# Attention of a fused kernel: the turns of queries and results through three PSUM banks in another order

## What is computed

```python
def phi(x):
    proj = np.einsum('bhsd,md->bhsm', x, omega)
    h = proj - np.sum(x * x, axis=-1, keepdims=True) / 2.0
    h = h - np.max(h, axis=-1, keepdims=True)
    return np.exp(h) / np.sqrt(m)
q_p, k_p = phi(q * scale), phi(k * scale)          # 4 x 8 heads, 576 x 128 each
kv = np.einsum('bhsm,bhsd->bhmd', k_p, v)
z = np.sum(k_p, axis=2)
num = np.einsum('bhsm,bhmd->bhsd', q_p, kv)
den = np.einsum('bhsm,bhm->bhs', q_p, z)[..., None] + 1e-06
attn_out = num / den
```

## Time and profile before

| | |
|---|---|
| median of 3 runs | 805.19 us (804.8 to 805.69) |
| profiled execution | 807.05 us, its span 805.2 us |
| TensorE, VectorE, ScalarE, GpSimd busy | 96%, 44%, 38%, 40% of the span |
| granted TensorE clock, mean | 0.992 |
| attention | the first 157 us |

### The profile page before, as it was taken

The page is one execution under the profiler, slowest core; times in us unless marked ns, Lnnn a source line. Parts: engine busy times, 40 slices in busy tenths (PEclk is TensorE's granted clock), DMA queues, the critical chain, the costliest instruction groups (busy, mean ns, idle before and its releaser), DMA issues.

```text
span 805.2 us, 15805 instructions
## 1 busy us (share of the span) xinstructions
PE 774.9 (96%) x5510; PEld 712.5 (88%) x5511; DVE 356.6 (44%) x908; ACT 308.9 (38%) x714; POOL 322.7 (40%) x280
## 2 busy tenths in 40 slices
PE   8899889999999999999999999999999999999994
PEld 7777778799899989988989998997999999999994
DVE  5777767511224424433442444666762322332221
ACT  3777776633232242232223224263224324425220
POOL 6777886135222222222222223243026726627421
PEclk9999999999999999999999999999999999999998
DMA  7876774011050020020002001141062532611111
GB/s 269 296 273 231 246 266 154 19 35 53 9 176 1 0 78 0 0 75 3 0 0 78 0 0 40 44 186 36 15 238 60 175 132 65 214 57 39 29 59 31
DMA packets 25732, 74.17 MB, mean 92 GB/s; under 512 B 3152, under 2 KB 4048, under 8 KB 25568
## 3 DMA queue, kind: packets, MB, share of 16 engines
q1 hardware_dynamic: 22432, 63.68, 22.7%
q0 software_dynamic: 3264, 10.03, 4.1%
HBM read 61.11 MB, written 12.58 MB: 92 GB/s over the span
## 4 chain that ended last, share of the span: by engine, by line
PE 88%; ACT 4%; DVE 3%; issue 3%; DMA 0%; ACTq 0%; POOL 0%; SPq 0%; POOLq 0%; DVEq 0%
PE pj L712 25%; PE nm L894 16%; PE pj L1312 8%; PE kv L894 8%; PE kv L1328 6%; PE nm L1328 6%; PE nm L1312 5%; PE pj L264 3%; PE kv L282 3%; ACT feat L427 2%; PE pj L1341 1%; PE tr L1299 1%; PE kv L313 1%; PE nm L340 1%; DVE pj L514 1%
## 5 line engine op out<-in xcount | busy, mean ns | idle before, releaser
L868 POOL TENSOR_TENSOR gl<-g,gh 128x384 fp32r<-128x384 f32 x96 | 100.9, 1053 | 304.7 <-ACT gh L730 304.7
L725 DVE TENSOR_TENSOR g<-pj,sg 128x384 f32<-128x384 f32 x96 | 53.5, 557 | 222.7 <-ACT sg L720 222.4
L720 ACT ACTIVATE sg<-pj 128x384 f32<-128x384 f32 x96 | 47.2, 491 | 253.3 <-PE pj L712 253.3
L712 PE MATMUL pj<-xh,win_h 128*128 128x384 f32 x384 | 129.6, 337 | 1.3 <-DVE xl L747 1.3
L712 PE MATMUL pj<-xh,win_l 128*128 128x384 f32 x384 | 129.5, 337 | 0.0
L712 PE MATMUL pj<-xl,win_h 128*128 128x384 f32 x384 | 129.0, 336 | 0.0
L712 PEld LDWEIGHTS pj<-xh,win_h 128*128 128x128 f32 x384 | 72.2, 188 | 5.2 <-DVE xl L747 1.5
L712 PEld LDWEIGHTS pj<-xl,win_h 128*128 128x128 f32 x384 | 72.1, 188 | 3.6
L712 PEld LDWEIGHTS pj<-xh,win_l 128*128 128x128 f32 x384 | 72.1, 188 | 0.0
L1312 PE MATMUL pj<-xTh,W 128*128 128x288 f32 x320 | 71.1, 302 | 0.0
L836 DVE SCALAR_TENSOR_TENSOR raw<-tr,xT 128x512 f32<-128x512 f32 x90 | 58.6, 688 | 8.2 <-DVE g L725 7.6
(11 more groups left out here) (255 smaller groups left out, 1691.1 us busy)
## 6 DMA issues: line engine op xcount, KB each, us to landing
wraw<-in_moe_w SPq DMA_DIRECT2D x7, 2048.0 KB, 10.8
ve<-in_v_z SPq DMA_DIRECT2D x16, 585.0 KB, 3.8
qk<-in_qk_n SPq DMA_DIRECT2D x15, 576.0 KB, 6.0
qkT<-in_qk_t SPq DMA_DIRECT2D x15, 576.0 KB, 6.8
y_rows<-ys SPq DMA_DIRECT2D x18, 256.0 KB, 2.4
stage<-in_moe_w_in SPq DMA_DIRECT2D x8, 512.0 KB, 7.1
y_early<-ys SPq DMA_DIRECT2D x12, 256.0 KB, 2.7
stage<-in_moe_w_out SPq DMA_DIRECT2D x4, 512.0 KB, 6.6
```

The costliest lines, as they stand in the source:

```text
L712: mm = eng.matmul(ph[f % 3][:, 0:BT], w[f // F1A][:, c, f % F1A, :], x[:, c, :], start=(c == 0 and w is win_h and x is xh), stop=(c == DC ...
L725: eng.tensor_tensor(g32[f % 2][:, :], ph[f % 3][:, 0:BT], sg[f % 2][:, :], ALU.mult).then_inc(v_g, 1)
L868: eng.tensor_tensor(gl[f % 3][:, :], g32[f % 2][:, :], gh[f % 3][:, :].bitcast(F32), ALU.subtract).then_inc(g_gl, 1)
```

## The change

The second query turn of each step goes into nm0, in all steps, and stands straight after the first, ahead of the third projection. The second result turn goes into nm1. The third query turn stands between the first and the second result turn. Waits follow the banks: the turn into nm0 waits for VectorE's quotient out of it, output 1 waits for the copy out of nm1, the sums no longer wait for a query copy. On ScalarE the exponentials b of group 1 move ahead of the copies of the result turns and of the third query turn, and the exponentials a of group 0 move from behind `copy_kv` to behind those copies: in even steps behind the exponentials b of group 2, just ahead of the other two a.

```diff
--- before.py
+++ after.py
@@ -276,27 +276,25 @@
             need(eng, a_kv, i)
             if a == 1 and not (isinstance(i, int) and i == 1):
                 need(eng, a_xs, 3 * n)
-            else:
-                need(eng, a_qf, 3 * i - 1)
             for j in range(RJ):
                 mm = eng.matmul(kv[:, 0:VW], feat[a][:, j, :], ve[a][:, j, :],
                                 start=(j == 0), stop=(j == RJ - 1))
             mm.then_inc(p_kv, 1)
 
-        def turn_qf(i, n, a, g, before):
+        def turn_qf(i, n, a, g):
 
             if g == 1:
                 eng.wait_ge(a_exa, PG * i + 3)
             else:
                 eng.wait_ge(a_exb, PG * i + 2 + g // 2)
 
-            if before or g == 0:
-                need(eng, a_qf, 3 * i + g)
+            if g == 0:
+                need(eng, a_qf, 3 * i)
             elif g == 1:
-                eng.wait_ge(a_kv, i + 1)
+                need(eng, v_nm, OG * (i - 1) + 1)
             else:
                 eng.wait_ge(a_qf, 3 * i + 1)
-            bank = kv if g == 1 and not before else tr
+            bank = nm[0] if g == 1 else tr
             for j in range(3):
                 mm = eng.transpose(bank[:, j * P:(j + 1) * P], feat[a][:, RJ + 3 * g + j, :], ident[:, :])
             mm.then_inc(t_qf, 1)
@@ -304,13 +302,14 @@
         def turn_x(n, g, unit):
 
 
+
             if g == 0:
                 eng.wait_ge(v_nm, 2 * OG * (n + 1))
                 eng.wait_ge(a_kv, unit + 1)
-            else:
-                eng.wait_ge(a_xs, 3 * n + g)
+            elif g == 2:
+                eng.wait_ge(a_xs, 3 * n + 1)
             for j in range(3):
-                mm = eng.transpose(kv[:, j * P:(j + 1) * P],
+                mm = eng.transpose((nm[1] if g == 1 else kv)[:, j * P:(j + 1) * P],
                                    xs[:, 3 * g + j, :, :].rearrange("p h d -> p (h d)"), ident[:, :])
             mm.then_inc(t_xs, 1)
 
@@ -327,13 +326,16 @@
                                    xs[:, 3 * g + j, :, :].rearrange("p h d -> p (h d)"), ident[:, :])
             mm.then_inc(t_xs, 1)
 
-        def output(i, n, a, t):
+        def output(i, n, a, t, before=False):
 
 
             lo, hi = O_GROUPS[t]
             eng.wait_ge(a_qf, 3 * i + (hi + 2) // 3)
             if t == 0:
                 eng.wait_ge(a_kv, i + 1)
+            elif before:
+
+                need(eng, a_xs, 3 * n - 1)
             need(eng, v_nm, OG * (i - 1) + t + 1)
             for j in range(lo, hi):
                 for b in range(2):
@@ -361,10 +363,10 @@
             before = a == 0 and not (isinstance(i, int) and i == 0)
             if last:
                 sums(i, n, a)
-                turn_qf(i, n, a, 0, before)
+                turn_qf(i, n, a, 0)
                 dense["up"](eng, 0, 0, (v_sb, PG * UNITS - 1))
-                turn_qf(i, n, a, 1, before)
-                turn_qf(i, n, a, 2, before)
+                turn_qf(i, n, a, 1)
+                turn_qf(i, n, a, 2)
                 dense["up"](eng, 0, 1, (a_exb, PG * UNITS - 1))
                 output(i, n, a, 0)
                 output(i, n, a, 1)
@@ -373,27 +375,28 @@
                     turn_last(g)
                 return
 
+
             project(*x, 0)
             project(*x, 1)
             sums(i, n, a)
-            turn_qf(i, n, a, 0, before)
+            turn_qf(i, n, a, 0)
+            turn_qf(i, n, a, 1)
             project(*x, 2)
             if before:
                 turn_x(n - 1, 0, i)
-            turn_qf(i, n, a, 1, before)
+            turn_qf(i, n, a, 2)
             if before:
                 turn_x(n - 1, 1, i)
-            turn_qf(i, n, a, 2, before)
-            if before:
                 turn_x(n - 1, 2, i)
             output(i, n, a, 0)
-            output(i, n, a, 1)
+            output(i, n, a, 1, before)
 
         half_steps(eng, step)
 
     def scalar(eng):
-        def copy_x(n, g, bank=kv):
-
+        def copy_x(n, g, bank=None):
+
+            bank = bank if bank is not None else nm[1] if g == 1 else kv
             eng.wait_ge(t_xs, 3 * n + g + 1)
             at = xT[:, :].rearrange("p (e b j c t) -> p e c j b t", e=2, b=2, j=RJ, c=DC)
             eng.activation(at[:, bass.ds(n // DC, 1), bass.ds(n % DC, 1), 3 * g:3 * g + 3, :, :]
@@ -401,9 +404,9 @@
                            bank[:, 0:3 * P].rearrange("p (j b t) -> p j b t", b=2, t=HD),
                            ACT.Copy).then_inc(a_xs, 1)
 
-        def copy_qf(i, n, a, g, before):
+        def copy_qf(i, n, a, g):
             eng.wait_ge(t_qf, 3 * i + g + 1)
-            bank = kv if g == 1 and not before else tr
+            bank = nm[0] if g == 1 else tr
             eng.activation(qfT[:, 3 * g:3 * g + 3, :].rearrange("p t c -> p (t c)"),
                            bank[:, 0:3 * P], ACT.Copy).then_inc(a_qf, 1)
 
@@ -439,10 +442,10 @@
             before = a == 0 and not (isinstance(i, int) and i == 0)
             if last:
                 copy_kv(i, n, a)
-                copy_qf(i, n, a, 0, before)
+                copy_qf(i, n, a, 0)
                 dense["sig"](eng, 0, 0)
-                copy_qf(i, n, a, 1, before)
-                copy_qf(i, n, a, 2, before)
+                copy_qf(i, n, a, 1)
+                copy_qf(i, n, a, 2)
                 dense["high"](eng, 0, 0)
                 dense["sig"](eng, 0, 1)
                 dense["high"](eng, 0, 1)
@@ -452,26 +455,26 @@
                 return
             exps_b(*x, 0)
             copy_kv(i, n, a)
-            exps_a(*x, 0)
-            copy_qf(i, n, a, 0, before)
+            copy_qf(i, n, a, 0)
+            copy_qf(i, n, a, 1)
+            exps_b(*x, 1)
             if before:
                 copy_x(n - 1, 0)
-            copy_qf(i, n, a, 1, before)
+            copy_qf(i, n, a, 2)
             if before:
                 copy_x(n - 1, 1)
-                copy_qf(i, n, a, 2, before)
-            exps_b(*x, 1)
-            if before:
                 copy_x(n - 1, 2)
             else:
-                copy_qf(i, n, a, 2, before)
-            exps_a(*x, 1)
+                exps_a(*x, 0)
             if isinstance(i, int) and i == UNITS - 2:
 
                 eng.wait_ge(g_sq, 4 * i)
                 eng.wait_ge(g_wl, NWIN + NWO)
                 dense["split_h"](eng, 0, 0)
             exps_b(*x, 2)
+            if before:
+                exps_a(*x, 0)
+            exps_a(*x, 1)
             exps_a(*x, 2)
             if isinstance(i, int) and i == UNITS - 2:
                 dense["split_h"](eng, 0, 1)
```

## The result

The changed kernel took 792.83 us in the median of 4 runs (790.65 to 793.36), the kernel before beside it 805.0 us (802.6 to 805.69): a ratio of 0.9849, with a 95% interval of 0.9834 to 0.9864. The forecast was 792.6.

The account below looks back on a forecast made before the run. Bound: TensorE's idle time in the chain turn, copy, next turn into the same bank. Savings of 11.6 + 1.3 + 0.3 - 0.6 = 12.6 us off 805.19 gave 792.6 us, range 789.3 to 797.0.

Parts of the forecast that it names:

- the chain turn, copy, turn: TensorE in the attention loop: each turn waits for the copy of the turn before in its bank; six rounds save 11.6 us.
- Projection 1's wait: TensorE in odd steps: projection 1 waits 0.35 us for the exponentials; the change was to remove this.
- The 0.23 that the forecast gives to the loop's branch: TensorE between output 1 and the next round: 0.23 us put down to the loop's branch, which stays.
- The 0.6 for register and wait instructions: In front of the new turns in the loop: added instructions cost 0.1 us a round, 0.6 us lost.
- GpSimd costed at nothing: Squares and loads in the loop: cover ahead of the norms falls from 2.9 to 0.9 us, so no time is lost.
- the forecast's own list of signs: Profile after: right if odd steps take 7.4 to 7.6; wrong if VectorE idles for GpSimd or odd steps exceed 7.9.
- rival B: Linked squares, low half, weight issue and load landing become the bound; landing of 8.6 loses 5.4 us: 798.0; chance 0.08.
- Step 14: End of attention: unit 15's sums start 1.1 us later, the dense product 0.2 to 0.4 earlier; 0.3 us gained.
- The sum: Whole kernel: 11.6 from six rounds, 1.3 from steps 0 and 1, 0.3 from step 14, less 0.6: 12.6 us.
- Rival A: ScalarE's copies in both steps come 0.5 us later after a later bias, costing 6.0 us: 798.6; chance 0.11.
- C: Rival, slower: load landings over 10.4 us eat the whole gain; at 11.0 the time is 807.6; chance 0.02.
- D: Rival: ScalarE's own load bounds the loop, not turn, copy, turn; rounds stay, time 805.2; chance 0.03.

## Why the prediction was right

**The chain.** The forecast rested on the chain turn, copy, turn in TensorE's gaps. Each bank undone brought its wait back, of the size worked out: without the second result turn's bank the even steps took 9.6 instead of 8.4, without the second query turn's a wait of 0.67 stood in each step. ScalarE's order alone gave 1.7 us of the loop, the banks alone 7.9, both 10.9 in the profile of the change.

**The steps.** Even 8.40 was forecast, 8.33 to 8.50 measured; odd 7.49, and 7.51 measured where nothing else waits, with 0.19 to 0.28 ahead of output 1 against 0.26 worked out. A round without GpSimd's waits is 95.5 / 6 = 15.9, forecast 15.89. Projection 1's wait went, as forecast. The unrolled step 1 fell from 7.85 to 7.14, 0.71 for 0.65. The 0.23 that the forecast gives to the loop's branch is not all the branch's: the next step starts 0.76 behind output 1 inside the loop (74.31 to 75.07) and 0.61 where no branch back is taken (122.31 to 122.92), so the branch is 0.15. It stands in both kernels and changes no difference.

**The 0.6 for register and wait instructions** is not borne out by the runs: with GpSimd's order altered the same instructions are there and the round is at 15.92. GpSimd filled the 0.6, and more: the loops of the change were 96.3, 96.9 and 98.4, 0.8 to 2.9 over 95.5.

**GpSimd costed at nothing** is the step that failed. That sentence of the forecast took the cover of the norms of one kind of unit, those read at 86.35 in an even step, 2.9 us, and left 0.9. The norms of the other kind, read in odd steps, follow squares that start only behind both low halves. Their cover was smaller (in the trace before, unit 8's squares ended at 75.9 and its norms were read at 77.8, so 1.9), and a round 1.9 shorter nearly used it up: 0.3 was left above. That is why it is the odd steps that grow; an even one grew once, by the late load. By the forecast's own list of signs one of wrong came beside those of right: VectorE idle ahead of the norms for GpSimd, and with it odd steps of up to 8.19 in the first profile where 7.4 to 7.6 were named. The ring of rival B was right as a mechanism, its longest landing of q and k too short: 9.3 came, where the rival put 8.6 and the argument against it 7.0. It cost that execution some 2 us, not 5.4, since it came once. Rival B's other argument, contention with VectorE, was not put to the test: while the squares ran, VectorE had no instruction with two inputs in SBUF (each of its two-input ones there reads pj or nm, which lie in PSUM), so their steady 2.10 to 2.12 says nothing for or against it.

**Step 14.** Sums at 10.35 forecast, 10.23 measured; the dense product at 12.9, and 12.56 measured. The 0.3 of gain was 0.55 there. But in one of the three profiles of the changed kernel, and in one of the two with the low half later, it was 14.2: the clock was at its lower level behind the new wait of 1.86 ahead of unit 15's sums, and 1.1 was lost against the kernel before in place of a gain. The forecast knew the wait and didn't ask what the clock would do behind it.

**The sum** came out because these are small and of both signs: the loop gave 8.9 to 10.9 for 11.0, steps 0 and 1 a little more than 1.3 (step 0, from its first query turn on, 3.37 instead of 4.19). That the time was met to 0.2 us is luck; the mechanism and the size of each step were not. Two figures of the forecast do not follow from its own sums: the lower bound comes to 789.7, and the range starts at 789.3; a landing of 8.0 gives 795.6, not 795.7. Neither matters for the result. Rival A did not occur: the bias left VectorE 5.3 after the start in both kinds of steps, as walked. C needed landings over 10.4; D is refuted by the two kernels that undid a bank.

## What to carry to other kernels

When a TensorE chain runs through a copy, give the next turn another bank and put a product of other data between a turn and what needs its copy; the place without the bank left 0.67 at every such turn here. Then look for cover by reader, not by engine: an engine that serves two kinds of steps has a cover for each, and the smaller one decides. Here the order of two GpSimd operations was worth 0.8 to 2.9 us of the loop once TensorE had become faster, while in the loop of the kernel before no norm waited at all. A wait that is moved to a place where little hangs on it may still be followed by a fall of the clock, as in some executions here.

## What the runs showed of the hardware

The granted clock fell to the lower level in some executions of one kernel and not in others, behind the same wait: TensorE stood idle 1.86 us in the profile of the change and of the later-low-half kernel's second run alike; in the first the 18 products of the sums took 2.25 at a clock of 1.00, in the second 3.90. Over the profiles of all kernels with this wait (1.85 or 1.86, eleven profiles) they took 2.25 in six, 3.06 in one and 3.90 in four; in the three profiles where TensorE was idle 0.62 or less there, 2.25 each time. What decides between them no run here shows. At the program's start, between 12 and 20 us, the clock was partly at the lower level in the profiles of the kernel before (0.77 in the stretch from 12 to 16) and of both repeats of the change (0.62 and 0.57 there), and at 1.00 in the first profile of the change; step 2 began at 30.65, 29.88, 28.02 and 26.60 in that order. So single profiles of this kernel are to be compared piece by piece: the loops of two profiles tell what their spans, here up to 2.2 us off the median on either side, don't.
